# Issuing the half-filled third contraction tile of a dense product as one pair on separate row halves of TensorE

## Time and profile before

| | |
|---|---|
| time, median of 3 runs (lowest, highest) | 420.82 us (420.04, 422.71) |
| the profiled execution: its own time | 417.85 us |
| the profiled execution: span, mean granted TensorE clock | 416.1 us, 0.984 |
| PE busy | 386.2 us, 93% of the span |
| DVE, ACT, POOL busy | 283.7, 225.9, 212.2 us |

### The profile page before, as it was taken

How to read it: one execution, slowest core, us unless ns; L and a number is a source line. 1 busy time by engine, 2 the same in 40 slices (tenths; PEclk the granted TensorE clock), 3 DMA queues, 4 the chain that set the end, 5 groups by cost and what they waited for, 6 DMA issues and landing times.

```text
span 416.1 us, 9463 instructions
## 1 busy us (share of the span) xinstructions
PE 386.2 (93%) x2741; PEld 359.5 (86%) x2742; DVE 283.7 (68%) x496; ACT 225.9 (54%) x406; POOL 212.2 (51%) x225
## 2 busy tenths in 40 slices
PE   0999996899999999999999999599999999999983
PEld 0858886789999999999999999588998999899873
DVE  8999989958656788557766676677473257874231
ACT  4647772454556545655555655546465358874230
POOL 6577978436556665342434464045264423886221
PEclk9999997899999999999999999989999999999998
DMA  7979774335255544644222254225736219741110
GB/s 198 304 286 320 231 221 147 112 83 165 76 182 172 184 134 153 189 135 166 72 71 61 66 202 143 105 64 174 277 117 260 64 40 354 262 153 36 56 36 26
DMA packets 30682, 63.43 MB, mean 152 GB/s; under 512 B 8984, under 2 KB 20763, under 8 KB 30012
## 3 DMA queue, kind: packets, MB, share of 16 engines
q1 hardware_dynamic: 28780, 57.61, 42.6%
q0 software_dynamic: 1808, 5.31, 3.8%
q10 hardware_dynamic: 64, 0.15, 0.1%
HBM read 56.40 MB, written 6.88 MB: 152 GB/s over the span
## 4 chain that ended last, share of the span: by engine, by line
PE 83%; DVE 8%; issue 2%; DMA 2%; ACT 2%; DVEq 0%; POOL 0%; SPq 0%; POOLq 0%; ACTq 0%
PE ps L1541 7%; PE ps L1543 7%; PE ps L1542 7%; PE ps L1525 5%; PE ps L1527 5%; PE ps L1526 5%; PE ps L1674 4%; PE ps L1676 4%; PE ps L1675 4%; PE ps L1631 3%; PE ps L1633 3%; PE ps L1632 3%; PE ps L1658 3%; PE ps L1532 3%; PE ps L1533 3%
## 5 line engine op out<-in xcount | busy, mean ns | idle before, releaser
L1156 DVE SCALAR_TENSOR_TENSOR gsum<-ps,soft 128x384 f32<-128x384 f32 x64 | 35.7, 557 | 51.8 <-ACT soft L897 51.5
L670 POOL TENSOR_TENSOR win_lo<-win_raw,win_hi 128x256 fp32r<-128x256 f32 x32 | 25.1, 783 | 85.6 <-DVE win_hi L1143 85.6
L889 ACT ACTIVATE soft<-ps 128x384 f32<-128x384 f32 x64 | 31.5, 492 | 68.5 <-PE ps L1533 68.4
L1541 PE MATMUL ps<-wout_hi,ghi 128*128 128x336 f32 x192 | 61.1, 318 | 1.0 <-DVE glo L1162 1.0
L1542 PE MATMUL ps<-wout_lo,ghi 128*128 128x336 f32 x192 | 60.7, 316 | 0.0
L1543 PE MATMUL ps<-wout_hi,glo 128*128 128x336 f32 x192 | 60.7, 316 | 0.0
L1525 PE MATMUL ps<-xhi,win_hi 128*128 128x384 f32 x128 | 43.6, 341 | 0.8 <-DVE gsum L1156 0.8
L1527 PE MATMUL ps<-xhi,win_lo 128*128 128x384 f32 x128 | 43.3, 338 | 0.0
L1526 PE MATMUL ps<-xlo,win_hi 128*128 128x384 f32 x128 | 43.2, 338 | 0.0
L1674 PE MATMUL ps<-split,hthi 128*128 x120 | 38.3, 319 | 1.9 <-DVE htlo L1333 1.9
L737 POOL DMA_INDIRECT out<-yout,token x15 | 17.7, 1177 | 41.3 <-DVE yout L1341 40.3
(11 more groups left out here) (214 smaller groups left out, 996.2 us busy)
## 6 DMA issues: line engine op xcount, KB each, us to landing
e1raw<-w_e SPq DMA_DIRECT2D x24, 512.0 KB
e2raw<-w_e SPq DMA_DIRECT2D x16, 640.0 KB, 5.2
win_raw<-w_in SPq DMA_DIRECT2D x32, 192.0 KB, 2.6
wout_raw<-w_out SPq DMA_DIRECT2D x32, 160.0 KB, 2.1
kq<-kq_t SPq DMA_DIRECT2D x16, 240.0 KB
wout_t<-w_out_t SPq DMA_DIRECT2D x3, 1024.0 KB, 14.1
og<-o_t SPq DMA_DIRECT2D x2, 1152.0 KB, 7.4
kr<-k_rows SPq DMA_DIRECT2D x8, 240.0 KB, 4.7
```

What stands on the lines that cost most here:

```text
L1156: dve.scalar_tensor_tensor(half(gsum, hf), ps[:, hf, 0:S // 2], 0.0, half(soft, hf), ALU.max, ALU.add).then_inc(g_done, 1)
L1541: pe.matmul(o, ghi[u][:, cols], wout_hi[u][:, :], start=False, stop=False, skip_group_check=True)
```

```diff
-        xlo = [keep.place(f"xlo{b}", [P, KT, S], F32R) for b in range(B)]
+        xlo = [keep.place(f"xlo{b}", [P, 2, S], F32R) for b in range(B)]
...
-        win_lo = [lay.place(f"win_lo{u}", [P, 2, P], F32R) for u in range(2)]
+        win_lo = [lay.place(f"win_lo{u}", [P, KT, P], F32R) for u in range(2)]
...
+def low_halves():
+
+    return ((slice(HALF, P), slice(0, S // 2)), (slice(0, HALF), slice(S // 2, S)))
...
+            def low_part_halves(b):
+                pool.wait_ge(xhi_done, KT * b + KT)
+                pool.wait_ge(wout_split, 4 * KT + 2)
+                for n, (rows, cols) in enumerate(low_halves()):
+                    pool.tensor_tensor(xhi[b][rows, 2, cols], xn[rows, 2, cols], xhi[b][rows, 2, cols].bitcast(F32), ALU.subtract).then_inc(xlo_done, 1)
+                    pool.wait_ge(xlo_done, X_LOW * b + 3 + n)
...
             def split_in(f, u):
                 pool.wait_ge(win_hi_done, f + 1)
-                pool.tensor_tensor(win_lo[u][:, :, :], win_raw[u][:, 0:2, :], win_hi[u][:, 0:2, :].bitcast(F32), ALU.subtract).then_inc(win_split, 1)
-
-                low = slice(HALF, P)
-                pool.wait_ge(win_split, 2 * f + 1)
-                pool.tensor_tensor(win_hi[u][low, 2, :], win_raw[u][low, 2, :], win_hi[u][low, 2, :].bitcast(F32), ALU.subtract).then_inc(win_split, 1)
+                pool.tensor_tensor(win_lo[u][:, :, :], win_raw[u][:, :, :], win_hi[u][:, :, :].bitcast(F32), ALU.subtract).then_inc(win_split, 2)
...
             def low_part(k):
                 dve.wait_ge(xhi_done, k + 1)
-                dve.tensor_tensor(xlo[0][:, k, :], xn[:, k, :], xhi[0][:, k, :].bitcast(F32), ALU.subtract).then_inc(xlo_done, 1)
+                if k < 2:
+                    dve.tensor_tensor(xlo[0][:, k, :], xn[:, k, :], xhi[0][:, k, :].bitcast(F32), ALU.subtract).then_inc(xlo_done, 1)
+                else:
+                    for rows, cols in low_halves():
+                        dve.tensor_tensor(xhi[0][rows, k, cols], xn[rows, k, cols], xhi[0][rows, k, cols].bitcast(F32), ALU.subtract).then_inc(xlo_done, 1)
...
             def hidden(b, f, u, first=False):
                 pe.wait_ge(win_split, 2 * f + 2)
                 hi, lo = win_hi[u], win_lo[u]
+                half = lambda hf: slice(hf * (S // 2), (hf + 1) * (S // 2))
+                o = [ps[:, hf, 0:S // 2] for hf in range(2)]
+                pe.wait_ge(g_done, 2 * f + 1)
                 for hf in range(2):
-                    pe.wait_ge(g_done, 2 * f + hf + 1)
...
-                    pe.matmul(o, hi[:, 2, :], xhi[b][:, 2, cols], start=False, stop=False)
-                    pe.matmul(o, hi[:, 2, :], xlo[b][:, 2, cols], start=False, stop=True).then_inc(h_ready, 1)
+                    last = pe.matmul(o[hf], hi[:, 2, :], xhi[b][:, 2, half(hf)], start=False, stop=(hf == 1), skip_group_check=True)
+                    if hf == 0:
+                        pe.wait_ge(g_done, 2 * f + 2)
+                        pe.matmul(o[0], lo[0:HALF, 2, :], xhi[b][0:HALF, 2, half(0)], start=False, stop=True, skip_group_check=True).then_inc(h_ready, 1)
+                        pe.matmul(o[1], lo[HALF:P, 2, :], xhi[b][HALF:P, 2, half(1)], start=True, stop=False, skip_group_check=True)
+                last.then_inc(h_ready, 1)
```

More of the change, by code:

```diff
@@ L50 @@
 SURE = TT
+X_LOW = KT + 1
+def low_halves():
+    return ((slice(HALF, P), slice(0, S // 2)), (slice(0, HALF), slice(S // 2, S)))
 def norm_pieces():
@@ L143, in build_program @@
         xhi = [keep.place(f"xhi{b}", [P, KT, S], F32R) for b in range(B)]
-        xlo = [keep.place(f"xlo{b}", [P, KT, S], F32R) for b in range(B)]
-        after_x = keep.at
+        xlo = [keep.place(f"xlo{b}", [P, 2, S], F32R) for b in range(B)]
         gat = Region(after_keep)
@@ L157, in build_program @@
         pick_1 = gat.place("pick_1", [P, HEADS], F32)
-        assert gat.at <= after_x
+        after_x = max(keep.at, gat.at)
         lay = Region(after_x)
@@ L408, in load_second @@
                 sp.dma_start(den[:, 1, :], nq_rows[H:2 * H, :].rearrange("h (p n) -> (h p) n", n=NQ)).then_inc(nq_loaded, 16)
-                sp.wait_ge(xlo_done, KT)
+                sp.wait_ge(xlo_done, X_LOW)
                 rows = attn_rows[DM:2 * DM, :]
@@ L697, in _ @@
                 split_step(i, 1)
-            with pool.Fori(1 + KT, 1 + 2 * KT) as i:
+            with pool.Fori(1 + KT, 2 * KT) as i:
                 split_step(i, 0)
@@ L702, in _ @@
                 low_part(1, i - 1 - KT)
+            split_step(2 * KT, 0)
+            normalise(1, KT - 1)
+            split_step(2 * KT, 1)
+            low_part_halves(1)
             def split2(r, halves=(0, 1)):
@@ L913, in sums @@
                 act.wait_ge(mm2_done, FT + FREE2)
-                act.wait_ge(xlo_done, B * KT)
+                act.wait_ge(xlo_done, B * X_LOW)
                 rows = slice(0, NC // 2)
@@ L1190, in sums @@
                 dve.wait_ge(mm2_done, FT + FREE2)
-                dve.wait_ge(xlo_done, B * KT)
+                dve.wait_ge(xlo_done, B * X_LOW)
                 rows = slice(NC // 2, NC)
@@ L1516, in hidden @@
                 hi, lo = win_hi[u], win_lo[u]
+                half = lambda hf: slice(hf * (S // 2), (hf + 1) * (S // 2))
+                o = [ps[:, hf, 0:S // 2] for hf in range(2)]
+                pe.wait_ge(g_done, 2 * f + 1)
                 for hf in range(2):
-                    pe.wait_ge(g_done, 2 * f + hf + 1)
-                    cols = slice(hf * (S // 2), (hf + 1) * (S // 2))
-                    o = ps[:, hf, 0:S // 2]
                     for k in range(2):
@@ L1524, in hidden @@
                             pe.wait_ge(xlo_done, k + 1)
-                        pe.matmul(o, hi[:, k, :], xhi[b][:, k, cols], start=(k == 0), stop=False)
-                        pe.matmul(o, hi[:, k, :], xlo[b][:, k, cols], start=False, stop=False)
-                        pe.matmul(o, lo[:, k, :], xhi[b][:, k, cols], start=False, stop=False)
+                        pe.matmul(o[hf], hi[:, k, :], xhi[b][:, k, half(hf)], start=(k == 0 and hf == 0), stop=False, skip_group_check=True)
+                        pe.matmul(o[hf], hi[:, k, :], xlo[b][:, k, half(hf)], start=False, stop=False, skip_group_check=True)
+                        pe.matmul(o[hf], lo[:, k, :], xhi[b][:, k, half(hf)], start=False, stop=False, skip_group_check=True)
                     if first and hf == 0:
                         pe.wait_ge(xhi_done, KT)
-                        pe.wait_ge(xlo_done, KT)
-                    pe.matmul(o, hi[:, 2, :], xhi[b][:, 2, cols], start=False, stop=False)
-                    pe.matmul(o, hi[:, 2, :], xlo[b][:, 2, cols], start=False, stop=True).then_inc(h_ready, 1)
+                        pe.wait_ge(xlo_done, X_LOW)
+                    last = pe.matmul(o[hf], hi[:, 2, :], xhi[b][:, 2, half(hf)], start=False, stop=(hf == 1), skip_group_check=True)
[4 more added lines that the diff above has]
+                last.then_inc(h_ready, 1)
             def second(f, u, last_tile):
@@ L1564, in _ @@
             pe.wait_ge(xhi_done, B * KT)
-            pe.wait_ge(xlo_done, B * KT)
+            pe.wait_ge(xlo_done, B * X_LOW)
             hidden(1, FT, 0)
```

## The result

| | time, median (lowest, highest) |
|---|---|
| before | 420.43 us (418.60, 422.71), 4 runs |
| changed | 427.99 us (424.96, 431.01), 4 runs |
| ratio | 1.0158, 95% interval 1.0106 to 1.0210 |

The ratio is clear of no change and holds the forecast's 1.016. In microseconds the interval is +4.5 to +8.8.

What follows compares the result with a forecast made beforehand. PE was taken to bound the dense stage, tile by tile. Visits less the saved slot +7.1 us, stalls -0.5, head +0.05 gave +6.7 us: 427.5 us on the median, 8-in-10 range 422.5 to 431.

Steps and rivals of the forecast that it cites:

- The slot saved: In `hidden` on PE, 14 full matmuls and a side-by-side pair replace 16 full ones: gain 0.176 us per tile, 5.6 us.
- The visits: On PE in each `hidden`, changing to row halves and back costs 0.40 us per tile, bounds 0 and 0.45.
- the faster rival: In `hidden`, changes of arrangement cost nothing, so the saved slot gains 5.4 us, to 415.4 us; chance 0.06.
- `second` at 2.77 us: PE's eighteen matmuls after `hidden` in each tile were to stay at 2.77 us.
- PE's stalls: Of about 0.8 us of PE waits after tile 1, part goes as DVE gets more time: -0.5 us, bounds 0 and -0.8.
- the shorter POOL work: POOL's two instructions per tile become one, 0.24 us less, beside PE with POOL half idle: effect on the time 0.
- The head: Before the dense stage's first tiles, DVE's third low part becomes two 384-column instructions instead of one of 768: +0.05 us.
- the forecast's own case: The forecast as summed, slower at 427.5 us on the median, 426 to 429.5 by its own bounds; chance 0.77.
- Gain after all: Rival for `hidden`: changes of arrangement cost nothing, a tile is 0.17 us shorter, -5.4 us, 415.4 us; chance 0.06.
- Half the price: Rival: only running-empty or only the bare weight load is paid, about 0.20 us for both visits, 421 to 424 us; chance 0.10.
- Not side by side: Rival: the pair's two matmuls take turns, another 0.176 us per tile, +12.3 us, 433 us; chance 0.07.
- The waits as the cause of the price: Semaphore waits on attention's pairs of heads might explain the 0.20 to 0.22 us leftover; the prediction rejected this.

Runs made afterwards that it cites:

- the two-pair kernel: Changed kernel with high and low weights both as pairs in one visit, the third tile's full matmul left out: 421.29 us, ratio 1.0009.
- the narrow kernel: Changed kernel with 64 weight columns instead of 128 in the pair and the second bank's wait at the start of `hidden`: 433.67 us, one run.
- the first experiment: Changed kernel with both low matmuls on all 128 rows, keeping mixed x tile, single POOL split and earlier wait: 420.46 us, ratio 1.0004.
- the batch-1 kernel: Changed kernel with the pair on row halves only in batch 1's sixteen tiles, batch 0 on the full array: 424.89 us, ratio 1.0130.
- the two-visit kernel: Changed kernel with the pair pulled apart, one half matmul mid-`hidden` and one at its end, each its own visit: 443.11 us, ratio 1.0559.

## Why the prediction held, step by step

**The slot saved** (0.176 us per tile): right. The pair starts within 0.01 us; on one row half it costs a slot more (3.21 us), alone nothing less (3.03).

**The visits** (0.40 us per tile, bounds 0 and 0.45): right, from the attention rows. In the changed kernel's tiles it is 0.39. That there are two parts each way, read there from a leftover, is shown by the two-pair kernel (four times 0.10). That one of them is the bare weight load is borne out by the loads' starts and by the narrow kernel (0.05 less for half the weight columns). That the other is the array running empty is my reading; no run takes it apart further. The Trainium skill's rule that a change of tiling mode drains the engine ("TensorEngine Tiling (Array Packing)", Tiling Modes) agrees with it: 0.27 us to the first matmul of the other arrangement instead of 0.18. It says nothing of a weight load that stands bare at the change, the other half of the price. The packing rule of the Trainium skill's "TensorE: Matmul & The Clock Gate", Part 3, on which the faster rival stood, fits inside a visit (the pair within 0.01 us) and not across its borders: by it alone the change would have gained 5.4 us. The Trainium skill's remark in the same Part 3 that weight loads overlap running matmuls only on other row groups, which the prediction set against that rival, is not what the trace shows: in the full-array stream each load starts beside the matmul before, on the same rows (96.03 for the matmul at 96.20). What stops it at the borders is the change of arrangement.

**`second` at 2.77 us**: nearly right. It is 2.80 and 2.77 in turn where it was 2.78 and 2.76, 0.015 us more in the mean. The kernel with the lone small matmul has it too, the one with everything on the full array and the one with both on one row half do not. Its cause stays open. With it a tile loses 0.233 us, not 0.22, which makes 7.5 us for 32 instead of 7.1.

**PE's stalls** (-0.5 us; it was -0.8, the end of its bounds): mis-sized, and for a reason that was in the main wrong. From tile 2 to 31 the tiles account for 29 x 0.233 = 6.8 us and the stretch grew by 5.96, so 0.8 us of stalls went, all there were. I put it to PE being slower. In the first experiment PE has its old pace, and tiles 13 and 14 are at 5.56 and 5.60 us without a stall; with POOL's split in two pieces they stall again at the same PE pace. So what was costed at 0, the shorter POOL work, was worth some 0.5 us of the 0.8 (163.58 against 163.05 us from tile 2 to 31). It came to 0.21 us per tile, 1.02 in place of 0.76 and 0.46, and the traces above suggest how: it moves POOL's long products away from DVE's casts. Tile 17's 0.2 us in `hidden`, ahead of the six extra matmuls, does go with PE's pace: it stays in the first experiment (3.01 us) and is gone with the pair.

**The head** (+0.05 us): mis-sized. From the second low part of x to the first matmul that needs the third went from 79.86 to 81.94, 2.08 us, to 82.14 to 84.41, 2.27: +0.19. I took the price of two 384-column instructions, 1.02 us, from the earlier trace rows; these two take 1.14, the second starting 0.59 us behind the first, where the 768-column one took 0.96.

**The sum**: 7.5 - 0.8 + 0.19 = 6.9 us, where the table of stretches has 6.8 and the forecast 6.7. Part of that nearness is luck: `second` and the head were too low by 0.4 and 0.14 us, the stalls' gain by 0.3. The range of the forecast's own case, "426 to 429.5", does not follow from its bounds either; they give 427.2 to 429.7. That the end follows PE tile by tile is borne out by the batch-1 kernel in its trace (half the tiles, half the loss), and by the two-visit kernel in its time too: 21.8 us more than before from tile 2 to 31, and 22.3 us more in the median.

**The rivals.** Gain after all: excluded. Half the price: excluded, all four parts of 0.10 are there. Not side by side: excluded. The waits as the cause of the price: excluded at the pair by the kernel with no wait there; the attention stage's leftover itself was not tested.

What stays open: whether the dense stage could run on row halves throughout, so that the visits vanish and fifteen slots stay (three products of 320 rows are 7.5 full slots per half of the tokens). Then both row halves would have to add to the same bank; it was not tried.

## What to carry to other kernels

In this kernel half-filled matmuls on separate row halves gave the full factor of two inside the pack, but a pack that stood alone in a stream of full matmuls paid for going in and coming out: 0.40 us against 0.176 us per pair. By these figures, an estimate, it takes three saved slots of 384 columns per visit to gain. Look for the price where the same kernel already changes arrangement: starts of neighbouring groups in the trace, less the matmuls themselves. PE's busy share hides it; the count of matmuls per stretch and the idle time of the weight loads show it.

## What the runs showed of the hardware that was not expected

A wait that is met just as the matmul could start was not free. Met 0.02 us ahead of the matmul's turn but 0.13 us behind the turn of its weight load, it cost 0.12 us in front and 0.08 us behind; over the tiles this made 434.43 us, in one run, out of the pair's 428.

Two 128 x 384 casts on DVE took 2.68 us while POOL ran a product of 768 columns beside them, against 0.62 us without one. With 0.21 us less POOL work per tile the mean cast was 433 ns in place of 596, in one trace of each. The Trainium skill's page "SBUF — State Buffer", section "SBUF: two separate sides", states that GpSimd and VectorE share one pair of ports, which a GpSimd instruction, or a VectorE one that needs the pair, holds for its whole length if it starts first, and the other waits. The 2.68 us of the casts beside the 1.96 us product agrees; that these casts are of the kind that needs the pair, no run here shows. An engine that is half idle is no free place for work if its instructions hold back another's.
